# Bits written ahead of the copy of scores, moves of x that wait for the sum of x, and the fourth weight slot split ahead of the x of the last heads

## What is computed

```python
q_bits = (np.einsum('bhsd,dk->bhsk', q, proj) > 0).astype(np.int64)
k_bits = (np.einsum('bhsd,dk->bhsk', k, proj) > 0).astype(np.int64)
mask = q_bucket[:, :, :, None] == k_bucket[:, :, None, :]
scores = np.where(mask, scale * np.matmul(q, k.transpose(0, 1, 3, 2)), -1000000000.0)
attn = np.exp(scores - np.max(scores, axis=-1, keepdims=True))
attn = attn / (np.sum(attn, axis=-1, keepdims=True) + 1e-09)
x = np.matmul(attn, v)                       # then (tokens, 512)
h = x @ w_in;  x = np.where(h > 0, h, np.exp(np.minimum(h, 0.0)) - 1.0) @ w_out
h = x @ w2_in; out = (s * np.maximum(h, 0.0) ** 2 + b) @ w2_out
```

## Time and profile before

| what | value |
|---|---|
| time, median of 3 runs | 790.07 us (789.47 to 790.96) |
| the profiled execution | 792.6 us, of which 790.8 us is the span from first to last instruction |
| TensorE busy | 755.7 us, 96% of the span |
| VectorE, ScalarE, GpSimd busy | 391.3, 315.5 and 309.7 us |
| mean granted TensorE clock | 0.982 |

### The profile page before, as it was taken

How to read it: one execution, slowest core, us unless ns; L and a number is a source line. 1 busy time by engine, 2 the same in 40 slices (tenths; PEclk the granted TensorE clock), 3 DMA queues, 4 the chain that set the end, 5 groups by cost and what they waited for, 6 DMA issues and landing times.

```text
span 790.8 us, 11790 instructions
## 1 busy us (share of the span) xinstructions
PE 755.7 (96%) x3760; PEld 648.9 (82%) x3760; DVE 391.3 (49%) x753; ACT 315.5 (40%) x612; POOL 309.7 (39%) x250
## 2 busy tenths in 40 slices
PE   8999799999899299999999999999999999999998
PEld 6998799889898188888888888888888888888886
DVE  5878588878685057434323433243233332242333
ACT  6888488888684021232222322232211222122121
POOL 5688689879796699100000166670000000000000
PEclk9999899999999699999999999999999999999999
DMA  5675654664521344100000033220000100010001
GB/s 157 144 160 142 132 129 124 144 146 124 114 60 41 89 134 133 53 1 1 1 0 1 0 107 98 88 80 1 1 1 9 44 0 0 0 53 0 0 0 53
DMA packets 44194, 50.67 MB, mean 64 GB/s; under 512 B 8244, under 2 KB 32644, under 8 KB 44164
## 3 DMA queue, kind: packets, MB, share of 16 engines
q1 hardware_dynamic: 43940, 50.06, 24.1%
q10 hardware_dynamic: 224, 0.22, 0.1%
HBM read 29.45 MB, written 3.19 MB: 41 GB/s over the span
## 4 chain that ended last, share of the span: by engine, by line
PE 76%; POOL 9%; issue 5%; DMA 5%; SPq 3%; DVE 1%; POOLq 0%; DVEq 0%
PE acc L649 33%; PE h_ps L631 32%; DMA x_parts<-x_second 3%; PE pt_ps L596 3%; PE s_ps L582 2%; POOL x_sum L445 2%; POOL pt_hi L426 2%; PE s_ps L583 2%; DMA qqk<-bits 1%; PE pv_ps L611 1%; PE pv_ps L612 1%; POOL pt_lo L428 1%; POOL xt_lo L450 1%; POOL x_sum L435 1%; POOL xt_hi L448 1%
## 5 line engine op out<-in xcount | busy, mean ns | idle before, releaser
L812 ACT ACTIVATE r_sb<-h_ps 128x512 f32<-128x512 f32 x96 | 57.4, 598 | 383.9 <-PE h_ps L631 383.9
L631 PE MATMUL h_ps<-xt_hi,wb_hi 128*128 (+1 forms) x288 | 112.0, 389 | 0.0
L631 PE MATMUL h_ps<-xt_lo,wb_hi 128*128 (+1 forms) x288 | 112.0, 389 | 0.0
L631 PE MATMUL h_ps<-xt_hi,wb_lo 128*128 (+1 forms) x288 | 112.0, 389 | 0.0
L843 DVE TENSOR_SCALAR_CACHE_REDUCE probs<-s_ps 128x768 f32<-128x768 f32 x96 | 91.8, 957 | 39.2 <-PE s_ps L583 36.8
L937 DVE SCALAR_TENSOR_TENSOR g_sb<-e_sb,h_ps 128x512 f32<-128x512 f32 x48 | 33.0, 688 | 151.4 <-ACT e_sb L815 150.9
L939 DVE TENSOR_SCALAR g_sb<-e_sb,sb_scale 128x512 f32<-128x512 f32 x48 | 27.8, 580 | 158.3 <-ACT e_sb L815 158.3
L741 ACT ACTIVATE probs<-probs,row_min 128x768 f32<-128x768 f32 x96 | 90.0, 937 | 3.7 <-DVE probs L843 3.0
L596 PE MATMUL pt_ps<-ident_sb,probs 128*128 128x128 f32 x576 | 81.2, 277 | 0.9 <-DVE pt_lo L850 0.9
L582 PE MATMUL s_ps<-kt,qqk 128*128 128x384 f32 x192 | 67.2, 350 | 13.9 <-DMA qqk<-qqk 7.1
L945 DVE TENSOR_TENSOR g_lo<-g_sb,g_hi 128x512 fp32r<-128x512 f32 x96 | 75.6, 787 | 3.3
(11 more groups left out here) (89 smaller groups left out, 1530.4 us busy)
## 6 DMA issues: line engine op xcount, KB each, us to landing
w_raw<-w_in_dram SPq DMA_DIRECT2D x32, 256.0 KB, 2.7
w_raw<-w_out_dram SPq DMA_DIRECT2D x32, 256.0 KB, 2.8
raw<-qk_dram SPq DMA_DIRECT2D x15, 384.0 KB, 5.3
qqk<-kt SPq DMA_DIRECT2D x15, 384.0 KB, 5.1
raw_v<-v_dram SPq DMA_DIRECT2D x16, 192.0 KB, 4.4
all_inv<-inv_dram SPq DMA_DIRECT2D x16, 192.0 KB
x_parts<-x_second SPq DMA_DIRECT2D x16, 192.0 KB, 7.5
out_dram<-o_sb SPq DMA_DIRECT2D x12, 256.0 KB, 2.1
```

The lines of the kernel that those rows point to most:

```text
L631: last = mm(bank[:], w[a][:, kt * P:(kt + 1) * P], x[b], start=n == 0, stop=n == 3 * KT - 1)
```

## The change

Four things are changed.

1. `write_bits` is issued at the start of units 0 and 6, ahead of `keep_x` and `keep_scores`, and no longer at their end (only the very first stays where it was). On SyncE `copy_bits` stands ahead of `copy_q_hi`.
2. `move_first` waits for `x_summed` and `get_inv` for `x_scaled`, where both waited for `x_split`.
3. The loads of slots 1, 2 and 3 go to pairs 2, 4 and 7, behind `put_inv(i, 1)`, where that of slot 0 is (pair 0). Before, slot 1 was loaded in the middle of pair 1, slot 2 at the end of pair 1, slot 3 behind all of attention.
4. GpSimd splits slot 3 ahead of `sum_x` and `split_x` of the last pair. On SyncE slot 4 is loaded between the last two `move_second`, and the last `get_inv` stands behind them.

```diff
+WEIGHT_PAIRS = (0, 2, 4, 7)
             def get_inv(i, n):
                 sp.wait_ge(inv_out[n], 32 * i + 32)
-                wait(sp, x_split, 2 * i - 1 + n)
+                wait(sp, x_scaled, 2 * i - 1 + n)
             def move_first(i, n):
-                wait(sp, x_split, 2 * i - 1 + n)
+                wait(sp, x_summed, 2 * i - 1 + n)
                 sp.wait_ge(x_done, GROUPS * i + n + 1)
...
                 copy_k(2 * i + 1)
+                copy_bits(2 * i + 1)
                 if nxt:
                     copy_q_hi(2 * i + 2)
-                copy_bits(2 * i + 1)
...
-                if i == 0:
-                    load_w(0, 0, 0, 0)
+                if i in WEIGHT_PAIRS:
+                    f = WEIGHT_PAIRS.index(i)
+                    load_w(0, f, f % 2, f - 1)
                 if nxt:
                     copy_k(2 * i + 2)
+                    copy_bits(2 * i + 2)
                     copy_q_hi(2 * i + 3)
-                    copy_bits(2 * i + 2)
...
-                if i == 1:
-                    load_w(0, 1, 1, 0)
...
-                    load_w(0, 2, 0, 1)
+            move_second(PAIRS - 1, 0)
+            load_w(0, EARLY, 0, EARLY - 1)
+            move_second(PAIRS - 1, 1)
             get_inv(PAIRS - 1, 1)
-            move_second(PAIRS - 1, 0)
-            move_second(PAIRS - 1, 1)
-            load_w(0, 3, 1, 2)
...
+            load_w(0, EARLY + 1, 1, EARLY)
...
+            weights(3)
             for n in range(2):
                 sum_x(PAIRS - 1, n)
                 split_x(PAIRS - 1, n)
-            weights(3)
...
+                if t == BITS_UNIT and (k < TILES or more) and not (first and k == 0):
+                    write_bits(2 * i + k // TILES + 1)
...
-                if t == BITS_UNIT and (k < TILES or more):
-                    write_bits(2 * i + k // TILES + 1)
+                if first and k == 0:
+                    write_bits(1)
```

More of the change, by code:

```diff
@@ L386, in _ @@
                     sp.dma_start(sb_scale[:, 1:2], b2.rearrange("(a n) -> a n", a=1).to_broadcast([P, 1])).then_inc(scale_in, 16)
-                    load_w(0, 2, 0, 1)
+            move_second(PAIRS - 1, 0)
+            load_w(0, EARLY, 0, EARLY - 1)
+            move_second(PAIRS - 1, 1)
             get_inv(PAIRS - 1, 1)
-            move_second(PAIRS - 1, 0)
-            move_second(PAIRS - 1, 1)
-            load_w(0, 3, 1, 2)
-            with sp.Fori(EARLY // 2, FT // 2) as j:
+            load_w(0, EARLY + 1, 1, EARLY)
+            with sp.Fori(EARLY // 2 + 1, FT // 2) as j:
                 for n in range(2):
```

## The result

The changed kernel takes **771.58 us** (median of 4 runs, 768.60 to 773.57) against 790.16 us for the kernel before on the same chip: ratio 0.976, 95% interval 0.972 to 0.980. Repeated later as `e1` it took 770.44 us, ratio 0.974 (0.972 to 0.977). It is faster by 18.6 us, where 30.6 were forecast, and lies outside the range of 757 to 767.

What follows compares the result with a forecast made beforehand. TensorE was busy 96% of the span, so only its waits and low clock could yield time. 16.1 us in attention plus 15.5 at the border, 31.6 off 790.07, gave 758.5; 759.5 was taken, leaving 1 us for small waits; range 757 to 767.

Steps and rivals of the forecast that it cites:

- 16.1 in attention: Heads' starts in attention: 12.0 us of TensorE waits for operands and 4.1 us of low clock behind them go.
- 15.5 at the border: Between attention and feed-forward: `hidden` of slot 4 begins at 265.4 instead of 280.95 us, 15.5 us less.
- The two are of one size, and I take 0: Loads in pairs 2 and 4: delay of 2.7 to 3.5 us behind them equals what `copy_bits` gains, net 0.
- Loads collide: Rival, loads in pairs 2 and 4: one wait of 1 to 3 us, perhaps low clock, 761 to 768 us; chance 0.17.
- If it lands as slowly as before, 5 us: Head's start: `copy_bits`, issued at about 162.7, lands at 167.7 against a need at 170.15, 2.4 us of slack.
- the queue is full because of the late `load_qk`: Heads' starts: late `move_first` holds back 384 KB of next q and k, which then travel just ahead of needed copies.
- the 36.1 us of `move_first`: SyncE's seven waits at `move_first` for the low part of x, together 36.1 us, forecast to fall to a few.
- The queue decides, not the issue: Rival: bits and k still land late, waits at heads' starts stay, only the border gains, 774.6 us; chance 0.06.
- the 7.1 us and the five: TensorE waits at heads' first scores: one of 7.1 us, five of together 4.9 us; all were to go.
- the stall that moves to slot 4: Stage border: the 14.9 us wait for slot 3 moves to slot 4 and shrinks to 1.1 us.
- A longer stall at slot 4: Rival, stage border: inverse or second half of x lands late, stall of 4 to 6 us, 763 to 766 us; chance 0.12.

Runs made afterwards that it cites:

- e13: Same kernel as `e5`, run again as yardstick, against the kernel before: 766.02 us, ratio 0.969.
- e5: The changed kernel with the loads of slots 1 and 2 moved to pair 6, against the kernel before: 763.7 us, ratio 0.966.
- e3: The changed kernel with `move_first` and `get_inv` waiting for `x_split` again, against the kernel before: 777.49 us, ratio 0.984.
- e11: `e5` with `move_first` and `get_inv` waiting for `x_split` again, against the kernel before: 774.93 us, ratio 0.978.
- e17: The changed kernel with the inverse read into 16 partitions instead of 128 from pair 1 on (x wrong), against the kernel before: 758.64 us, ratio 0.959.
- e10: `e5` with bits written behind the copy of scores and moved behind `copy_q_hi` again, against the kernel before: 765.99 us, ratio 0.967.
- e14: `e5` with the inverse read into 16 partitions instead of 128 from pair 1 on (x wrong), against the kernel before: 759.23 us, ratio 0.960.
- e18: `e5` reading 48 of 384 numbers of the inverse into all 128 partitions from pair 1 on (x wrong), against the kernel before: 758.7 us, ratio 0.959.
- e9: `e5` with `get_inv(i-1, 1)` behind the second `move_second` and `put_inv(i, 1)` behind `load_v(2i+3)` on SyncE, against the kernel before: 768.0 us, ratio 0.971.
- e12: The changed kernel with the same move of `get_inv` and `put_inv(i, 1)` on SyncE as `e9`, against the kernel before: 768.71 us, ratio 0.970.
- e2: The changed kernel with the loads of slots 1 and 2 back in pair 1, against the kernel before: 768.92 us, ratio 0.974.

## Why the prediction was wrong

The forecast was 31.6 us from two sums, 16.1 in attention and 15.5 at the border, less 1. Measured are 6.7 in attention and 12.8 at the border, and 2.4 in the start-up, which no term held.

**The step that failed is the third edit, "The two are of one size, and I take 0".** Measured: 5.8 us in pair 2, and 4.5 to 6.6 us in the whole by `e13` and `e5` against `e1`. The rival *Loads collide* had this mechanism with 0.17, and 761 to 768 as its time; the measured time lies above that too, since a second loss comes on top. What I set against the delay was the gain of `copy_bits`. But k stands behind the same 512 KB and has gained nothing: it lands at 89.96 us, 0.2 before bits, so TensorE would have waited for k alone. `copy_k(6)` takes 8.2 us to land, where it takes 3.7 in `e5` without the load, and it is issued 2.0 us later (81.72 us against 79.74). Timeline of SP in pair 2:

```profile
76.37 0.55 SPq L334 DMA_DIRECT2D x_parts<-x_second  x1
80.27 0.33 SPq L314 DMA_DIRECT2D inv_dram<-row_inv  x1
80.65 0.43 SPq L306 DMA_DIRECT2D w_raw<-w_in_dram  x1
81.13 0.50 SPq L307 DMA_DIRECT2D w_raw<-w_out_dram  x1
81.72 0.49 SPq L290 DMA_DIRECT2D kt<-kt  x1
82.31 0.86 SPq L296 DMA_DIRECT2D qqk<-bits  x1
83.23 0.64 SPq L277 DMA_DIRECT2D qqk<-kt  x1
```

`put_inv` waits until 80.27 for the read of the inverse, so `copy_k` goes 3.5 us behind the signs of 78.23, with 512 KB ahead of it.

**The second step that failed is "If it lands as slowly as before, 5 us", and under it "the queue is full because of the late `load_qk`".** The order of issue became what I forecast: the 36.1 us of `move_first` are gone, `e3` and `e11` show that this was worth 7 to 9 us, and in pair 5 `copy_bits(11)` is issued early, at 153.73 us. But it takes 7.4 us to land, and `copy_bits(13)` 8.2. In the kernel before, `move_first(4, 1)` and `load_qk` went some 5 us behind the read of the inverse, and `move_first` landed in 2.1 us, `copy_k` in 3.5 (medians of all). Now `move_first(i, 1)` goes 0.7 us behind the read, and the medians are 6.3 and 5.6. So edit 2 moved work to where two of the engines are held, and I had taken the landing times of the old places. A part of the 5.0 us lost in pairs 5 to 7 is this, and reaches TensorE by way of bits and of GpSimd; `e17`, where these moves land soon, loses nothing there. The rival *The queue decides, not the issue* had this part with 0.06; its 774.6 us took all of attention's gain away, and 6.7 us of it came. I used a number that spoke of the cause: 7.0 us for the inverse's 192 KB, while 256 KB land in 2.7. I took it as a price and did not ask why it was so long.

**Right:** the waits that edits 1 and 2 aim at (the 7.1 us and the five) go, once the read of the inverse is short, in `e17` for all pairs. There the whole sum can be seen: 758.64 us against 791.28 before, 32.6 us less, of which 2.0 are the start-up (sign matmuls at 24.45 us), so 30.6 where 31.6 were worked out. That the two agree so well is in part luck, since the inverse in `e17` is also quicker than in the forecast. Right too are the stall that moves to slot 4, and that the loads of slots 4 and 5 do no harm there. Edit 1 has a larger part in the prediction than `e10` shows for it: what it earns is mostly the start-up, which nobody forecast.

**Mis-sized, the border:** 14.3 us and then 1.5 of low clock, where 15.5 were forecast. The stall is 2.4 us, not 1.1. No DMA is late there. From the first cast of slot 3 to the end of slot 4's low part GpSimd takes 16.2 us (241.23 to 257.41) where my rows gave 3.55 + 7.80 + 3.55 = 14.9. The excess is in the eight steps on x, 9.2 us (244.69 to 253.87) instead of 7.80. Timeline of POOL, then of DVE:

```profile
244.69 1.20 POOL L436 TENSOR_TENSOR x_sum<-x_parts 128x384 f32<-128x384 f32 x1
246.03 1.39 POOL L446 TENSOR_TENSOR x_sum<-x_sum,all_inv 128x384 f32<-128x384 f32 x1
...
248.15 1.34 POOL L451 TENSOR_TENSOR xt_lo<-x_sum,xt_hi 128x384 fp32r<-128x384 f32 x1
...
255.07 2.34 POOL L471 TENSOR_TENSOR wb_lo<-w_raw,wb_hi 128x1024 f32 x1 [0.17 <-POOL wb_hi L469]
```

```profile
243.35 1.68 DVE L946 CAST g_hi<-g_sb 128x512 fp32r<-128x512 f32 x1
245.06 1.38 DVE L948 TENSOR_TENSOR g_lo<-g_sb,g_hi 128x512 fp32r<-128x512 f32 x1
...
255.21 2.74 DVE L948 TENSOR_TENSOR g_lo<-g_sb,g_hi 128x512 fp32r<-128x512 f32 x1
```

The sum took 0.99 us in the earlier trace rows, when VectorE was idle; here it takes 1.20, beside VectorE's splits of g. `g_lo` in turn takes 2.74 us beside `wb_lo`, and 0.82 in the mean of its 96. With the feed-forward's first work moved up beside x of the last pair, the two engines meet. The Trainium skill (SBUF — State Buffer, SBUF: two separate sides) says that a GpSimd instruction that reads SBUF and a VectorE instruction with two SBUF inputs need a common pair of ports. The one that starts first has it for the whole instruction, and the other one blocks. The trace agrees: `wb_lo` starts first, at 255.07, and `g_lo` ends at 257.95, 0.5 us behind `wb_lo`'s end at 257.41. No run separates this, so the 1.3 us are put down to it by timing alone.

**Clock.** The forecast took no loss behind a stall of about 1 us. The stall was 2.4 us, and the clock behind it 0.50, which cost 1.5 us. That differs from one execution to the next: in `e1` the same stall of 2.4 us has 1.00 over the 3.5 us behind it. Behind stalls of 1.85 us at this place it was 0.55 in `e5` and 1.00 in `e17`. In attention it was 0.50 behind the wait of 2.6 us, and 1.00 from 176.4 to 186.4 us with waits of 0.6 and 0.3.

One number of the prediction was read wrong: the two moves of the rival *A longer stall at slot 4* took 8.75 us (253.65 to 262.40), not 8.6. Nothing else rests on it.

**Open.** `e14`, `e17` and `e18` also let SyncE and GpSimd go on sooner, since the inverse lands sooner. How the gain of 7 to 12 us divides between copies that wait for two engines and SyncE's standing is not shown; `e9` and `e12` don't tell, as they also moved the read. In pair 2 the standing has a part: in `e17` `copy_k(6)` is issued at 80.01 us, 1.7 earlier. `e2` has the same reads, and the two late shares too (2.6 and 4.1 us for `copy_k(11)`), but less late, and no head waits in its pairs 3 to 7; what keeps it ahead there is not shown. And the read of all 192 KB spread over 16 engines, as two moves with 64 partitions outermost, was not tried. By the above it should bring the changed kernel near the 759 us of `e17` with nothing left out, as an estimate: on 16 engines the two reads are 1.0 us of 27 on each.

## What to carry to other kernels

A mean DMA share of 0.6 doesn't say that there is room: look at one transfer in a quiet stretch, and divide its share by 1/16 to get the engines it runs on. The updates of a move's semaphore show the rest: most early and two late means that two engines are held. A move that lands two times slower than a larger one is a question to be asked before its time is used as a price. When a load is moved within a queue, price every copy that stands behind it at the moment of its need, not only the one that the change speeds up. When a move is issued earlier, its old landing time is no price for the new place. A wait for several semaphores may carry the name of one that nobody needed: compare its landing with the time at which the engine went on. And if waits wander from pair to pair when one is removed, it is a resource that is short and not an order that is wrong.

## What had not been expected

- A broadcast read of 192 KB on 2 of 16 DMA engines, 49 GB/s, some 4.0 us twice a pair, and the last two shares of the moves behind it 3 to 6 us late. Shortening it took 7 us off one version and 12 us off another (0.974 to 0.959), more than moving the loads did.
- VectorE's `g_lo` of 128x512 takes 2.74 us beside GpSimd's `wb_lo`, against a mean of 0.82.
- Writing bits early pays in the start-up: 2.4 us here, 3.6 by `e10` against `e5`.
